# A fused attention and two-layer feed-forward kernel: the tiles that straddle two batches computed from raw float32 operands

## The reference

```python
def sm_attn(qq, kk, vv):
    s = scale * np.matmul(qq, kk.transpose(0, 1, 3, 2))
    a = softmax(s)                      # rows, with 1e-9 in the denominator
    return np.matmul(a, vv)
p_packed = sm_attn(p, k, v)             # 8 batches, 8 heads, 32 packed rows, 64 wide
out = sm_attn(q, p_packed, p_packed)    # 8 batches, 8 heads, 576 rows
x = out, tokens by heads*64             # 4608 x 512
h = x @ w_in                            # 4608 x 1024
ln = layernorm(h * softmax(h)) * g_ln
y = ln @ w_out                          # 4608 x 512
h2 = max(y @ w1, y @ w2, y @ w3)        # 4608 x 768
result = h2 @ w_out2                    # 4608 x 512
```

## Time and profile before

| | |
|---|---|
| median of 3 runs | 1035.26 us (1034.15 to 1037.35) |
| the profiled execution | 1035.78 us, span 1034.0 us |
| TensorE busy | 1001.0 us, 97% of the span |
| VectorE, ScalarE, GpSimd busy | 609.7, 348.4, 269.0 us |
| blocks 2 to 8 of stage 2 | 203.4 to 465.5 us, 36.3 or 39.0 us each |
| first matmul of stage 3 | 488.73 us |

### The profile page before, as it was taken

One profiled execution on the slowest core, in us unless ns is written; L12 is line 12 of the kernel. 1 busy time (PEld: TensorE's weight loads), 2 busy tenths in 40 slices (PEclk: granted clock), 3 DMA queues, 4 the chain that ended last, 5 costly groups with the idle time before them and its releaser, 6 DMA issues.

```text
span 1034.0 us, 14973 instructions
## 1 busy us (share of the span) xinstructions
PE 1001.0 (97%) x6050; PEld 806.9 (78%) x6050; DVE 609.7 (59%) x984; ACT 348.4 (34%) x559; POOL 269.0 (26%) x228
## 2 busy tenths in 40 slices
PE   7997789999999999999999999999999999999998
PEld 5655458788888888887888888888888888888887
DVE  2888889856665678556466636656355725553021
ACT  4766544433433424324122332214122331223111
POOL 0368652957947585600000000000000000000000
PEclk9999999999999999999999999999999999999999
DMA  8988734346443363215754435543546345442351
GB/s 283 387 276 293 260 129 169 102 165 219 171 165 144 140 231 123 82 63 208 289 210 165 185 121 195 214 170 126 182 184 214 146 159 182 175 153 92 112 163 41
DMA packets 47269, 183.17 MB, mean 177 GB/s; under 512 B 8160, under 2 KB 8160, under 8 KB 37600
## 3 DMA queue, kind: packets, MB, share of 16 engines
q1 hardware_dynamic: 40976, 147.21, 40.2%
q0 software_dynamic: 6224, 35.00, 8.9%
HBM read 134.62 MB, written 47.58 MB: 176 GB/s over the span
## 4 chain that ended last, share of the span: by engine, by line
PE 81%; DVE 11%; ACT 4%; issue 3%; POOL 1%; DMA 0%; ACTq 0%; DVEq 0%
PE ps L1133 28%; PE ps L766 26%; PE ps L1165 14%; PE ps L1156 5%; PE ps L1035 2%; PE ps L875 1%; ACT a L1237 1%; DVE h_lo L1525 1%; DVE spot L1847 1%; DVE bn L1714 1%; DVE packedT L1585 1%; PE ps L780 1%; DVE spot L1838 1%; DVE a2T L1620 1%; POOL a L668 1%
## 5 line engine op out<-in xcount | busy, mean ns | idle before, releaser
L1133 PE MATMUL ps<-ys,slot 128*128 128x512 f32 x1512 | 346.1, 390 | 0.6
L1133 PEld LDWEIGHTS ps<-ys,slot 128*128 128x128 f32 x1512 | 283.2, 188 | 62.8 <-ACT spot L1208 3.9
L1838 DVE TENSOR_TENSOR spot<-ps,spot 128x512 f32<-128x512 f32 x108 | 74.3, 688 | 104.6 <-PE ps L1133 75.4
L1208 ACT ACTIVATE spot<-ps 128x512 f32<-128x512 f32 x90 | 52.8, 596 | 208.1 <-PE ps L1133 197.1
L766 PE MATMUL ps<-ln_lo,w_out_s_hi 128*128 128x512 f32 x280 | 109.0, 389 | 0.0
L766 PE MATMUL ps<-ln_hi,w_out_s_lo 128*128 128x512 f32 x280 | 109.0, 389 | 0.0
L766 PE MATMUL ps<-ln_hi,w_out_s_hi 128*128 128x512 f32 x280 | 108.9, 389 | 0.0
L1165 PE MATMUL ps<-w_out_s_lo,h_hi 128*128 128x512 f32 x216 | 84.0, 389 | 0.0
L1165 PE MATMUL ps<-w_out_s_hi,h_hi 128*128 128x512 f32 x216 | 84.0, 389 | 0.0
L1165 PE MATMUL ps<-w_out_s_hi,h_lo 128*128 128x512 f32 x216 | 84.0, 389 | 0.0
L1341 ACT ACTIVATE u<-ps,neg_max 128x1024 f32<-128x1024 f32 x36 | 40.2, 1118 | 126.0 <-DVE neg_max L1696 126.0
(11 more groups left out here) (158 smaller groups left out, 1488.5 us busy)
## 6 DMA issues: line engine op xcount, KB each, us to landing
slot<-w_operands SPq DMA_DIRECT2D x36, 1792.0 KB, 7.2
w_operands<-stage POOLq DMA_DIRECT2D x18, 1024.0 KB, 4.9
v_raw<-in_v_dram SPq DMA_DIRECT2D x8, 1152.0 KB, 6.3
q_raw<-in_q_dram SPq DMA_DIRECT2D x32, 288.0 KB, 5.1
y_features<-yst SPq DMA_DIRECT2D x9, 1024.0 KB, 4.4
y_raw<-y_features SPq DMA_DIRECT2D x9, 1024.0 KB, 5.3
out_dram<-spot SPq DMA_DIRECT2D x36, 256.0 KB, 2.1
slot<-w_operands SPq DMA_DIRECT2D x9, 1024.0 KB, 5.1
```

What stands on the lines that cost most here:

```text
L1133: last = pe.matmul(ps[:, group_bank(g, k), :], w[:, a - 1, i, kk, :], ys[:, b, j, kk, :], start=n < 4 and kk == 0 and e == 0, stop=kk == K ...
L1208: return act.activation(dst, src, ACT.Copy)
L1838: dve.tensor_tensor(dst[:, :], a, b, op).then_inc(ready, 1)
```

## The change

For n > 9 (tiles 13, 22 and 31) the straddling tile is no longer made of four split terms. The raw float32 values are loaded anew from `m_dram` and `a_dram` into `straddle_m` (128 x 2 x 2 x 1024, both batches) and `straddle_a` (64 columns each), which lie where `w_out2_s` lies, and h is made by 8 plain float32 products: two quads, two halves of 512 columns, and for each the first batch to partitions 0 to 63 and the second batch to partitions 64 to 127 (128 x 64 weights, 512 columns moving). w_out2 can be split only when the last of these tiles is made, so it moves behind GpSimd's last `block_scale`, and SyncE waits for it before `load_slot(0)`.

```diff
+    straddle_m = place_at(cursor[0] - 2 * K2 * DM * 4, "straddle_m", [P, 2, QUADS, FF1])
+    straddle_a = place_at(cursor[0] - 2 * K2 * DM * 4 + 2 * QUADS * FF1 * 4, "straddle_a", [P, 2, QUADS, TAIL])
...
+            def load_straddle(q):
+
+                if q > 1:
+                    sp.wait_ge(h_filled, 9 * (q - 1) + 5)
+                for x in range(2):
+                    at = slice(S - TAIL, S) if x == 0 else slice(0, TAIL)
+                    sp.dma_start(straddle_m[:, x, :, :], m_dram[2 * q + x]).then_inc(straddle_loaded, 16)
+                    sp.dma_start(straddle_a[:, x, :, :], a_dram[2 * q + x][:, :, at]).then_inc(straddle_loaded, 16)
...
                     load_y(0, 0)
+                    sp.wait_ge(a_stored, 16 * (B - 2))
+                    load_straddle(1)
+                elif t in (3, 5):
+                    load_straddle((t + 1) // 2)
             for t in range(6, BLOCKS - 1):
                 store_y(t)
 
             sp.wait_ge(w_stored[0], 16 * GROUPS)
             sp.wait_ge(w_stored[1], 16 * GROUPS)
+            sp.wait_ge(w_out2_split, K2 // 2)
             load_slot(0)
...
             for n in range(2):
-                load_piece(n)
+                load_operands(n)
             block_scale(0)
-
-            wait_alone(pool, a_stored, 16 * (B - 2))
-            wait_alone(pool, m_stored, 16 * (B - 2))
-            wait_alone(pool, t_filled, 1)
-            for n in range(W2_END):
-                split_piece(n)
             s = 0
             for t in range(1, BLOCKS):
                 block_scale(t)
                 for _ in range((0, 1, 2, 1, 1, 2, 1, 1, 0)[t]):
                     split_operands(s)
                     s += 1
+            for n in range(2):
+                load_w_out2(n)
+
+            wait_alone(pool, h_filled, 9 * 3 + 5)
+            for n in range(K2 // 2):
+                split_w_out2(n)
+                if n + 2 < K2 // 2:
+                    wait_alone(pool, w_out2_split, n + 1)
+                    load_w_out2(n + 2)
...
-                if batch < 2:
+                if n > 9 and len(terms) > 1:
+                    pe.wait_ge(straddle_loaded, 64 * (n // 9))
+                elif batch < 2:
...
+                if n > 9 and len(terms) > 1:
+
+                    for g in range(QUADS):
+                        for w in range(WIDE):
+                            for x in range(2):
+                                last = pe.matmul(ps[half(x), bank + w, :], straddle_a[:, x, g, :],
+                                                 straddle_m[:, x, g, w * 512:(w + 1) * 512],
+                                                 start=g == 0, stop=g == QUADS - 1)
+                    last.then_inc(h_filled, 1)
+                    return
                 three_passes([(ps[:, bank + w, :],
...
                 pe.wait_ge(h2_split, base + parts * (MH - 1))
+                if t == 0:
+                    pe.wait_ge(w_out2_split, K2 // 2)
```

More of the change, by code:

```diff
@@ L243, in packed_attention_ffn @@
     in_loaded = [sem(f"in_loaded{i}") for i in range(2)]
+    straddle_loaded, w_out2_loaded = sem("straddle_loaded"), [sem(f"w_out2_loaded{i}") for i in range(2)]
+    w_out2_hi, w_out2_split = sem("w_out2_hi"), sem("w_out2_split")
     in_hi, in_split = sem("in_hi"), sem("in_split")
@@ L283, in packed_attention_ffn @@
     thirds = [w.rearrange("(k p) (m i n) -> p k m i n", p=P, m=2, n=P) for w in (w1, w2, w3)]
[L284 to L287, removed]
     def raw_operands(n):
@@ L293, in raw_count @@
     def raw_count(n):
-        return sum(16 if c < W2_END else 32 for c in range(n % 2, n + 1, 2))
+        return 32 * (n // 2 + 1)
     def rows(t):
@@ L575, in _, with load_operands @@
             wait_alone(pool, gain_loaded, 16)
[L577 to L583, removed]
+            def load_operands(n):
+                i, w = divmod(n, 3)
                 dst = weight_raw[n % 2][:, :].rearrange("p (m k n) -> p m k n", m=2, n=P)
@@ L586, in load_piece, with load_w_out2, split_w_out2 @@
                     pool.dma_start(dst[:, 1 - m, :, :], thirds[w][:, :, m, i, :]).then_inc(raw_loaded[n % 2], 16)
[L588 to L598, removed]
+            def load_w_out2(n):
+                dst = weight_raw[n % 2][:, :].rearrange("p (k n) -> p k n", k=2)
+                pool.dma_start(dst, w_out2_v[:, 2 * n:2 * n + 2, :]).then_inc(w_out2_loaded[n % 2], 16)
+            def split_w_out2(n):
+                hi, low = (w[:, 2 * n:2 * n + 2, :] for w in w_out2_s)
+                raw = weight_raw[n % 2][:, :].rearrange("p (k n) -> p k n", k=2)
+                wait_alone(pool, w_out2_loaded[n % 2], 16 * (n // 2 + 1))
+                pool.tensor_scalar(hi, raw, 1.0, None, ALU.mult).then_inc(w_out2_hi, 1)
+                wait_alone(pool, w_out2_hi, n + 1)
+                pool.tensor_tensor(low, raw, hi.bitcast(F32), ALU.subtract).then_inc(w_out2_split, 1)
             def split_operands(s):
-                n = W2_END + s
+                n = s
                 raw = raw_operands(n)
@@ L624, in split_operands @@
                 pool.dma_start(w_dram[s][:, 0:4], stage[:, 0:4, :, :, :].bitcast(F32)).then_inc(w_stored[0], 16)
-                if n + 2 < W2_END + GROUPS:
-                    load_piece(n + 2)
+                if n + 2 < GROUPS:
+                    load_operands(n + 2)
                 pool.wait_ge(sums_step, 4 * s + 4)
```

## The result

The changed kernel takes 1050.28 us (median of 4 runs, 1046.52 to 1050.39) against 1035.15 us before: a ratio of 1.0133, 95% interval 1.0114 to 1.0152. It is slower by 1.3%, clear of the spread of the runs. The profiled execution took 1050.29 us with a span of 1048.5 us, 14.5 us more than the earlier trace rows.

The account below looks back on a forecast made before the run. TensorE was taken to bound the kernel (busy 1001.0 of 1034.0 us). Forecast: 1035.8 - 5.4 (products) - 2.1 (block 1) + 12.6 (first stall) + 7.9 (end of stage 2) + 3.2 (clock) = 1052.0 us, range 1044 to 1058.

Parts of the forecast that it names:

- both loads in time: Rival: straddle landed at 242.4 and w_out2 split by about 476, only gains left, 1028.3 us; chance 0.05.
- The products: Tiles 13, 22, 31: plain float32 products take 3.7 instead of 5.5 us a tile, -5.4 us for three.
- upper bound, 6.9 us: Straddling tile's cost if its two column parts ran one after the other: 16 passes of 0.43 us.
- Mode changes: Switching TensorE between full array and column parts: little cost; at 0.2 us a change the sum would be 0.6 us higher.
- Block 1: w_out2's split leaves GpSimd there, VectorE speeds up, TensorE's waits of 1.4 and 0.7 us go: -2.1 us.
- The first stall: TensorE waits at tile 13 for the first straddle load, queued behind load_y(0, 0) on SyncE: +12.6 us, bounds 10 and 16.
- the landing at 255.0: Time the first straddle load lands, its last third slowed by GpSimd's stores and loads from 248 on.
- earliest: Earliest landing of load_y and straddle, 3200 KB in one queue: 241.45 + 2.6 + 3.1 x 2.7 = 252.4.
- The end of stage 2: Late w_out2 split, done at 484.0, delays slot 0 and load_y(0, 1); stage 3 starts at 496.6, not 488.73: +7.9 us.
- the prediction's sign: Expected in the changed trace: TensorE idles about 8 us ahead of L1133, released by VectorE's ys.
- rival of late loads: End of stage 2: GpSimd's w_out2 loads land after 8.1 us instead of 5, split done 488.1, +4, 1056 us; chance 0.15.
- The clock: TensorE's granted clock halves for 3 us after each of two idle times, about 1.6 us each: +3.2 us, bounds 0 and 6.

Follow-up runs that it names:

- one part alone: Second column part's products left out of tiles 13, 22 and 31, against the version with straddle load and w_out2 split both early: 1027.94 us, one execution.
- the moved split alone: All tiles as in the kernel before the change, with only w_out2's loads and splits moved ahead of block_scale(8): 1032.77 us, ratio 0.9971.

## Why the prediction was right, and where its terms were off

The direction and size came from two waits read out of the order of two queues, and both are shown: each goes away alone when its step is moved (1036.05 and 1041.52 us), and together they leave 1028.9 us, within 0.6 us of the 1028.3 that the rival "both loads in time" gave as its price. The time, 1050.28, is 1.7 us below the forecast of 1052.0. That it is so near is partly luck: the profiled execution had about 2 us in stage 1 that no term names. Of the four runs one took 1046.52 us; without a trace of it, it isn't shown whether stage 1 made the difference.

- **The products**: 3.7 us a tile was forecast, 3.6 measured from the first pass to the next matmul; the gain of 1.8 a tile came out as 1.64 in the block times, 4.9 us for three instead of 5.4. The part that the row with four parts didn't show, that two parts of 64 columns overlap as well, holds fully (one part alone takes as long as two). The upper bound, 6.9 us, wasn't reached even with the parts one after the other (5.35).
- **Mode changes**: they cost about 0.4 us a tile for both changes. The first pass starts 0.32 us after the last full-array matmul (341.38 to 341.70) where two matmuls are 0.227 apart, the bunch takes 3.58 us against 3.4 for eight rounds, and the second full-array matmul behind it comes after 0.34 us (421.62 to 421.96). These small distances outside the 3.6 us are most of the difference between a gain of 1.9 and the measured 1.64. The drain that the Trainium skill names (TensorEngine Tiling (Array Packing), Key Properties) is there at most in this size, and the 0.2 us a change, which the prediction worked out beside it and took up only in part, was about right.
- **Block 1**: 2.1 us forecast, 2.57 in the table and 2.6 by the moved split alone. So the bound, that no more than the two waits could be gained, was half a microsecond too strict.
- **The first stall**: 12.6 us forecast, 10.04 measured. The mis-sized step is the landing at 255.0: GpSimd's stores did not slow it by what load_in(4) had suffered. The 3200 KB landed 11.3 us after the first issue, near the "earliest" of the working (11.0).
- **The end of stage 2**: 7.9 us forecast, 7.65 measured, but by another road: TensorE idles 1.6 us ahead of the first matmul of stage 3, where the prediction's sign was about 8. The split took 22.3 us from the first load's issue to its end (468.53 to 490.87) where 22.4 was worked out, and y(0, 1) landed at 500.70. What the working missed is that VectorE and ScalarE, slowed beside GpSimd, hold TensorE for 4.0 us earlier, at `down(8, 2)`. As the slot's chain ends later anyway, this took part of the same stall and didn't add to it; with the split moved ahead, both are gone. The Trainium skill (SBUF — State Buffer, SBUF: two separate sides) describes a lock in which the loser of the shared port waits for the whole instruction. Three of VectorE's records agree with it: they end at 479.06, 485.76 and 491.42 us, each 0.55 or 0.56 us behind the end of a tensor_tensor of GpSimd (478.50, 485.20, 490.87). Two don't: that of 478.98 takes 2.77 us instead of 1.22 and that of 485.68 takes 1.52 instead of 0.69, and both end in the middle of a tensor_scalar of GpSimd; what slowed them stays open. The prediction had put a second rule beside its rival of late loads: by the Trainium skill (the same section) GpSimd can't write a DMA's descriptors while VectorE holds the shared port. The section says this of VectorE's 2-port modes, and VectorE ran tensor_tensor here, so the prediction's "by that rule this rival holds" went too far. The rival did not come: the first two loads, issued with VectorE idle, landed after 4.2 and 5.5 us, the third, issued beside its work, after 4.1; 5 had been taken.
- **The clock**: 3.2 us forecast, 2.5 measured (the remainder in block 3), all of it at tile 13. At the end of stage 2 the clock did fall, but while the slot's chain was still under way: the low stretch at 489 to 493 us (0.57 in the windows above) lay on the last `down` products, ahead of the wait for ys, and cost nothing.
- **Stage 1**: +1.96 us up to up(1, 1), in no term of mine. Two executions of one and the same kernel differ by 3.17 us at this point, so the spread of executions is enough to explain it; what decides it stays open.

The sum was nearer than its terms: the first stall was 2.6 us too high, the clock 0.7, and stage 1 took 2.0 of that back. The errors of the products and of block 1, half a microsecond each, cancelled.

## What to carry to other kernels

When an edit adds a load, find its place in the issuing queue and the time at which the instruction ahead of it may go, and compare that with the time at which its reader starts: here the queue's order alone (242 against 242.4) decided, and moving the same four DMAs 35 us up turned a loss of 1.3% into nothing. When a step is moved to the end of a queue because its buffer comes free later, ask whether it must stand behind everything or only behind what frees the buffer; GpSimd had 20 idle us ahead of `block_scale(8)`, and the same work there cost nothing. Both moves together made it 0.6% faster than the kernel before. Of these 6.4 us some 2.6 to 2.9 come from taking the split out of block 1, which needs no new products; the raw float32 tiles themselves are worth 3.9 to 4.8 us.

When two versions differ by a few microseconds, compare their traces from a point behind the stage that varies by itself: here three differences of medians lay 0.8 to 1.7 us off what had been worked out, and the same differences from up(1, 1) on lay within 0.3 us.

## What was not expected of the hardware

Matmuls on two column parts overlap even when they are not issued in turn. With all passes of one part ahead of the other's, the tile took 5.35 us instead of 6.9, and the doubled rounds lie in its middle: the first four passes of the second part start beside the last four of the first, so ahead of passes that were issued earlier. Between column parts "every engine runs its instructions in order" is therefore not exact for TensorE. With four passes of each part in a row nearly all overlapped (3.64 against 3.58 us). Why it is four isn't shown. And a wait of 5.5 us slowed tile 13 as much (6.62 us instead of 3.65) as one of 10 us (6.07).
